# A chain of attention and two gated MLPs on one core: TensorE's blocks of 512 columns put in two runs of three per group

## What is computed

```python
attn_out = _attn_ref(q, k, v)            # pooled attention, repeated 4 times, + windowed attention
x = transpose(attn_out) -> (2304, 512)
# first MLP, d_ff 1536
x = (sigmoid(x @ w_gate) * (x @ w_val)) @ w_out
# second MLP, d_ff 2048
h = x @ w_in
out = (h * sigmoid(1.702 * h)) @ w_out2
```

## Time and profile before

| | |
|---|---|
| median of 3 runs | 907.33 us (904.14 lowest) |
| profiled execution | 904.31 us, of which the span is 902.6 us |
| granted TensorE clock over the span | 0.998 |
| PE busy | 890.5 us, 99% of the span, 6566 matmuls |
| DVE / ACT / POOL busy | 57% / 53% / 77% |
| DMA | 80.39 MB, mean 89 GB/s |
| matmuls of 512 columns (L403, layer 2) | 864 |
| matmuls of 384 columns (L413, L415, L416 and L403 in layer 1) | 3384 |

### The profile page before, as it was taken

The page is one execution under the profiler, slowest core; times in us unless marked ns, Lnnn a source line. Parts: engine busy times, 40 slices in busy tenths (PEclk is TensorE's granted clock), DMA queues, the critical chain, the costliest instruction groups (busy, mean ns, idle before and its releaser), DMA issues.

```text
span 902.6 us, 17597 instructions
## 1 busy us (share of the span) xinstructions
PE 890.5 (99%) x6566; PEld 831.7 (92%) x6566; DVE 514.7 (57%) x960; ACT 482.0 (53%) x964; POOL 694.1 (77%) x547
## 2 busy tenths in 40 slices
PE   8989899999999999999999999999999999999998
PEld 6878799999999999998989999999998898989987
DVE  5767545455555555556565455555655656565565
ACT  5777655455444455454555455544555554545442
POOL 5779789999778999778786679998777877565641
PEclk9999999999999999999999999999999999999999
DMA  9866112222222222222212122422222221232111
GB/s 337 257 218 211 43 47 70 71 71 71 70 72 70 70 71 71 70 71 71 70 54 86 48 71 70 141 71 71 70 71 70 69 72 48 93 117 80 38 47 70
DMA packets 26580, 80.39 MB, mean 89 GB/s; under 512 B 2944, under 2 KB 2944, under 8 KB 26496
## 3 DMA queue, kind: packets, MB, share of 16 engines
q1 hardware_dynamic: 26496, 79.28, 27.4%
HBM read 74.55 MB, written 4.72 MB: 88 GB/s over the span
## 4 chain that ended last, share of the span: by engine, by line
PE 98%; issue 1%; ACT 1%; DMA 0%; DVE 0%; SPq 0%
PE o_ps L403 39%; PE d_ps L413 7%; PE d_ps L415 7%; PE d_ps L416 7%; PE s_ps L413 6%; PE s_ps L415 6%; PE s_ps L416 6%; PE t_ps L415 3%; PE t_ps L416 3%; PE t_ps L413 3%; PE o_ps L376 1%; PE o_ps L396 1%; PE t_ps L388 1%; PE t_ps L349 1%; PE d_ps L328 1%; PE d_ps L336 1%
## 5 line engine op out<-in xcount | busy, mean ns | idle before, releaser
L1148 DVE TENSOR_TENSOR att<-o_ps,att 128x512 f32<-128x512 f32 (+1 forms) x246 | 152.9, 625 | 150.6 <-PE o_ps L403 150.6
L1341 POOL TENSOR_TENSOR w_lo<-w_sum,w_hi 128x1024 fp32r<-128x1024 f32 x60 | 144.4, 2406 | 65.6 <-ACT w_hi L709 65.6
L1336 POOL TENSOR_TENSOR w_lo<-w_raw,w_hi 128x768 fp32r<-128x768 f32 x60 | 110.7, 1846 | 27.2 <-ACT w_hi L705 27.2
L415 PE MATMUL d_ps<-xs_lo,w_hi 128*128 128x384 f32 x360 | 120.5, 335 | 0.0
L413 PE MATMUL d_ps<-xs_hi,w_hi 128*128 128x384 f32 x360 | 120.4, 335 | 0.0
L416 PE MATMUL d_ps<-xs_hi,w_lo 128*128 128x384 f32 x360 | 120.4, 334 | 0.0
L1354 POOL TENSOR_TENSOR v_lo<-v_raw,v_hi 128x1024 fp32r<-128x1024 f32 x42 | 101.0, 2404 | 23.3 <-ACT v_hi L713 23.3
L1315 POOL TENSOR_TENSOR w_sum<-w_raw 128x256 f32<-128x256 f32 x120 | 88.5, 738 | 38.9 <-PE t_ps L416 28.7
L403 PE MATMUL o_ps<-v_hi,g_lo 128*128 128x512 f32 x288 | 114.0, 396 | 0.0
L403 PE MATMUL o_ps<-v_lo,g_hi 128*128 128x512 f32 x288 | 113.6, 394 | 0.0
L403 PE MATMUL o_ps<-v_hi,g_hi 128*128 128x512 f32 x288 | 111.9, 389 | 0.0
(11 more groups left out here) (120 smaller groups left out, 2049.4 us busy)
## 6 DMA issues: line engine op xcount, KB each, us to landing
v_raw<-in_w_out_dram SPq DMA_DIRECT2D x42, 512.0 KB, 3.5
w_raw<-in_w_gate_val_dram SPq DMA_DIRECT2D x36, 512.0 KB, 3.5
w_raw<-in_w_in_dram SPq DMA_DIRECT2D x24, 512.0 KB, 3.5
vw<-in_v_win_dram SPq DMA_DIRECT2D x16, 390.0 KB, 4.4
vt<-in_v_tok_dram SPq DMA_DIRECT2D x16, 320.0 KB, 4.3
qk<-in_q_t_dram SPq DMA_DIRECT2D x16, 288.0 KB, 4.2
qk<-in_k_t_dram SPq DMA_DIRECT2D x16, 288.0 KB, 5.3
out_dram<-att SPq DMA_DIRECT2D x18, 256.0 KB, 4.4
```

The lines of the kernel that those rows point to most:

```text
L415: pe.matmul(bank, wh[:, w, cols], xl[:, x, c, :], start=False, stop=False, skip_group_check=True)
L1148: vec.tensor_tensor(part, value, part, ALU.add).then_inc(y_added, 1)
L1336: gp.tensor_tensor(w_lo[b % 2][:, A11:A22 + 1, :], w_raw[b % 2][:, R11:R22 + 1, :], w_hi[b % 2][:, A11:A22 + 1, :], ALU.subtract).then_inc ...
L1341: gp.tensor_tensor(w_lo[b % 2][:, S1:S4 + 1, :], w_sum[b % 2][:, S1:S4 + 1, :], w_hi[b % 2][:, S1:S4 + 1, :], ALU.subtract).then_inc(ws_re ...
```

## The change

Only the order of the calls in two transitions changes, on three engines. PE does the five products p1, p2, p6, p5, p7 one after the other, then blocks 0, 1, 2, then p4 and p3, then blocks 3, 4, 5. `from_two_to_one` does the same and then the five products of the second set. ScalarE's and VectorE's lists are reordered so that their work comes in the order in which PE now makes it. No instruction, wait, buffer or size is added or removed.

```diff
--- before.py
+++ after.py
@@ -544,37 +544,37 @@
             def from_two_to_two(k):
                 n = FIRST[k + 1]
                 p1(n)
-                second(k, 0)
                 p2(n)
                 p6(n)
-                second(k, 1)
                 p5(n)
                 p7(n)
+                second(k, 0)
+                second(k, 1)
                 second(k, 2)
                 p4(n)
+                p3(n)
                 second(k, 3)
-                p3(n)
                 second(k, 4)
                 second(k, 5)
 
             def from_two_to_one(k):
                 n, w = FIRST[k + 1], LAST[k + 1]
                 p1(n)
-                second(k, 0)
                 p2(n)
                 p6(n)
-                second(k, 1)
                 p5(n)
                 p7(n)
+                second(k, 0)
+                second(k, 1)
                 second(k, 2)
                 p4(n)
+                p3(n)
                 second(k, 3)
-                p3(n)
+                second(k, 4)
+                second(k, 5)
                 p1(w)
-                second(k, 4)
                 p2(w)
                 p6(w)
-                second(k, 5)
                 p5(w)
                 p7(w)
 
@@ -871,11 +871,11 @@
                 snap_u2(n)
                 hi11(k + 1)
                 next_first_sums(k)
-                round_out(k + 1)
                 snap_u3(n)
                 sig22(k + 1)
+                round_out(k + 1)
+                hi22(k + 1)
                 round_x_step(k)
-                hi22(k + 1)
                 sig21(k + 1)
                 hi21(k + 1)
                 sig12(k + 1)
@@ -885,16 +885,16 @@
                 n, w = FIRST[k + 1], LAST[k + 1]
                 snap_p1(n)
                 round_in(w)
-                round_in_sums(w)
                 sig11(k + 1)
                 snap_u2(n)
-                round_out(k + 1)
+                round_in_sums(w)
                 snap_u3(n)
                 sig22(k + 1)
+                round_out(k + 1)
                 sig21(k + 1)
                 sig12(k + 1)
+                next_first(k)
                 snap_p1(w)
-                next_first(k)
                 snap_u2(w)
                 hi11(k + 1)
                 next_first_sums(k)
@@ -1203,37 +1203,37 @@
 
             def from_two_to_two(k):
                 n = FIRST[k + 1]
-                add_up(k, 0)
                 c11(n)
                 gate11(k + 1)
-                add_up(k, 1)
                 low11(k + 1)
                 c22(n)
+                add_up(k, 0)
+                gate22(k + 1)
+                add_up(k, 1)
+                low22(k + 1)
                 add_up(k, 2)
-                gate22(k + 1)
-                add_up(k, 3)
                 gate21(k + 1)
-                low22(k + 1)
                 c12(n)
                 low21(k + 1)
+                add_up(k, 3)
+                gate12(k + 1)
                 add_up(k, 4)
-                gate12(k + 1)
+                low12(k + 1)
                 add_up(k, 5)
-                low12(k + 1)
 
             def from_two_to_one(k):
                 n, w = FIRST[k + 1], LAST[k + 1]
+                c11(n)
+                c22(n)
                 add_up(k, 0)
-                c11(n)
                 add_up(k, 1)
-                c22(n)
                 add_up(k, 2)
+                c12(n)
                 add_up(k, 3)
-                c12(n)
                 add_up(k, 4)
+                add_up(k, 5)
                 c11(w)
                 gate11(k + 1)
-                add_up(k, 5)
                 low11(k + 1)
                 c22(w)
```

## The result

The changed kernel takes a median of 903.80 us over 22 runs, the kernel before 905.66 us over 22 runs beside it. The ratio is 0.9977 with a 95% interval of [0.9968, 0.9987]: faster by 0.13 to 0.32%, 2.1 us by the ratio. One run of each kernel lies far outside the others (1463.9 us before, 1248.4 us after) and the ratio leaves both out.

A forecast was written before the change was run, and what follows sets the result against it. PE, busy 890.5 of 902.6 us, was taken as the bound. From the profiled 904.3 us, 1.2 us came off for fewer width changes (1.1 over 22 transitions, 0.05 for the other), giving 903.1 us, range 901.3 to 907.0.

The forecast's parts named there:

- What bounds the kernel: In the MLPs PE goes matmul to matmul; only start distances or new waits move time; one late release cost about 0.3 us.
- The price by place: Second MLP transition: 0.20 us excess over settled distances, at width changes; entering a run of three blocks costs 41 ns.
- The exit of a run of three: Product behind three 512-column blocks: 34 ns chosen, between 4 and 60; gain 51 ns a transition, 1.1 us over 22.
- the nearest row: Trace row for leaving a run of two blocks: p1 took 1.07 us in place of 1.04, 26 to 30 ns.
- Free moves on the other engines: Reordered ScalarE, VectorE and GpSimd work costs nothing if PE finds each release in time; four close covers named.
- One spare: Time between snap_p1's end at 1.74 and p6's load due at 1.95 us in a transition: 0.21 us.
- The price of a miss: If one of the four covers fails, each miss costs its lateness and about 0.1 us more.
- The rule against it: Skill's spacing N / 2.4 + 2.5 ns, by column count alone; no order could be better and the sum would be 0.
- Rival 1: No gain, 904.3 us: excess belongs to the blocks, not width changes, or leaving a long run costs 60 ns; chance 0.2.
- Rival 2: Leaving a long run in the second MLP is cheap, 4 ns, giving 901.7 us; chance 0.07.
- Rival 3: p6 and p7 wait for ScalarE's copies in all 23 transitions, 0.15 us each product, 910 us; chance 0.1.
- The median: Whole kernel: a measured median can stand up to 3 us above what the program itself does.

The follow-up runs named there:

- e4: Changed kernel with ScalarE's rounding of the output weights put back ahead of snap_u3; median 908.86 us, ratio 1.0035 to the kernel before.
- e5: Changed kernel with a spare ScalarE copy of 192 columns ahead of snap_p1 in the second MLP; ratio 1.0010 to the kernel before.
- e3: Separate kernel, TensorE alone: runs of 6 to 36 wide matmuls, each followed by 36 narrower; 512 among 384 cost 30 ns for six, 60 to 70 for others.
- e1: Changed kernel with all six 512-column blocks in one run in 21 of 22 transitions; ratio 0.9957 to the kernel before, changed part 502.34 us.
- e2: Changed kernel with the six blocks in three runs of two per transition; ratio 0.9999 to the kernel before, changed part 505.20 us.

## Why the prediction was right

The forecast was 903.1 us with a range of 901.3 to 907.0; 903.80 was measured, and the forecast gain of 1.2 us stands beside 1.51 in the trace and 2.1 [1.2, 2.9] by the ratio. That the total came within 0.7 us is partly luck: the sum started from one execution of 904.31 us, 1.35 us under the median of 22 runs of the kernel before, and the gain was taken too small, and the two errors point opposite ways. The range also took in no change at all, so it is the distances in the trace that test the mechanism, not the total.

- *What bounds the kernel.* Held. PE goes from matmul to matmul in the changed part, before and after, but for one late release of the kind in the earlier trace rows, at the end of the second `from_one_to_two`, which costs about 0.30 us in both. Only the distances moved.
- *The price by place.* Held: the entry of a run of three is 41 ns as taken from the last blocks, and the excess of 201 ns a transition became 2 x (41 + 26) = 134.
- *The exit of a run of three.* The one unknown term. I took 34 ns, it is 26, the value of the nearest row; the "little for what the six matmuls did not show" was not there, since the sixth, at 0.18 us, is the last unsettled one. This is the 0.3 us by which the gain was undersized: 22 x 67 ns and about 0.07 for the one other transition make 1.54 us, and 1.51 was measured.
- *Free moves on the other engines.* Held in the outcome. e4 shows that one of them, the rounding of v behind snap_u3, was necessary, by the chain named. One spare was misjudged: for p6 the hand-over from ScalarE takes 0.11 us (e5), not 0.05. p7's load too begins 0.19 us after its copy's end in the changed kernel, so if the hand-over is the same there, which no run tested, it has 0.08 us as well. The loads of blocks 2 and 5 begin 0.26 us after their additions' ends, where 0.24 was worked out.
- *The price of a miss.* Wrong, though nothing in the sum hung on it. It was put at the lateness and about 0.1 us more. Every late release measured cost less than its lateness: 0.30 us for 0.36 in the kernel before, 0.26 for 0.33 inside the run of e4, 0.11 for 0.15 in e5.
- *The rule against it.* In e3 a bfloat16 matmul of 384 columns took 162.5 ns and one of 512 columns 216, with no dependence on place; in rounded float32 the same kernel took 173.3 and 226.6 ns, with it. The rule of the Trainium skill in "TensorE: Matmul & The Clock Gate", section "Back-to-back issue gap" (N / 2.4 + 2.5 ns), agrees with the bfloat16 figures and not with the others. The section calls this the gap of an isolated matmul and gives about 131 ns a matmul at 512 columns for a sustained stream; no run here shows a distance that short.
- *Rivals.* Rival 1, that the excess belongs to the blocks, is ruled out by the changed kernel's own transition (15.57 us, and 26 ns on leaving in place of 60), and e1 and e2 agree. It had been given 0.2 because two runs of one cost as much as one of two; that equality is real and ends there. Rival 2 (exit 4 ns) is ruled out by the same 26 ns. Rival 3 (waits in front of p6 and p7) did not happen but was closer than written: 0.08 us more on the copy would have started it, though by the prices of e5 it would have cost less than the 0.15 us a product that was put on it.
- *The median.* The note that a measured median may stand some microseconds off the sum was right: in the profiled executions the changed part repeats and what varies lies ahead of the first transition in question, by 3.4 us.

## What to carry to other kernels

When an engine is busy without a gap, look at the distance between starts by place, and not at mean durations: here only that showed what an order can be worth, and it is small, 0.2 us in 15.6. Where two widths of rounded float32 matmuls alternate, count the price for each length of run from the trace before grouping them: grouping one block to two gained nothing, and only from there on did each joined run pay. And when an order on one engine is changed for such a gain, write down the time of each release that gets close and fit the other engines' lists first; one rounding at its old place cost three times what the new order brings.

## What was not expected of the hardware

- The price of a change of width is not a fixed one: 34 ns for a run of 6 matmuls of 512 columns among 384, 67 ns for 12, 18, 24 or 36; 20 ns at any length among 256; and among 448, from the run of 12 on, the 36 narrow matmuls behind each run were 4 ns each faster than behind the run of 6 (7.29 in place of 7.42 us). Both distances last to the end of the 36. In bfloat16, measured with 512 among 384 alone, no price showed. The cause is open.
- Rounded float32 matmuls settle 13.3 ns above their columns at 2.4 GHz at 256, 384 and 512 columns (120.0, 173.3, 226.6 ns), at 448 columns 20 ns (206.7); bfloat16 ones 2.5 ns (162.5 and 216 ns).
- A release by a copy on ScalarE reached TensorE's weight load 0.11 us after the copy's end (e5), one by an addition on VectorE after 0.05 us (the kernel before, e4).
- The changed part repeated within about 0.01 us in two executions (503.73, 503.72), while the unchanged start took 392.69 to 396.10 us in the seven profiled executions with the same order up to there. From the first output block to the first p1 it is 263.81 to 263.87 us in all seven, so nearly all of that spread lies before the first block, in the attention stage and the first products.
